# Attention, MLP and routed experts on one core: the routing tables behind the MLP in another order

## The reference

```python
attn = attention(q, k, v)          # B=2, H=8, S=768, D=64; 8 global keys and a local window of 96, ALiBi bias
x = attn.transpose(0, 2, 1, 3).reshape(1536, 512)
h = x @ w_in                       # 512 -> 2048
x = (np.maximum(h, 0) + alpha * np.minimum(h, 0)) @ w_out

logits = x @ w_gate + modality_bias[modality_id]      # 8 experts
e_idx = np.argmax(logits, axis=1)
probs = softmax(logits); gate_w = probs[np.arange(N), e_idx]
for e in range(8):
    mask = e_idx == e
    h = np.maximum(x[mask] @ w1[e], 0.0)              # 512 -> 1024
    out[mask] = gate_w[mask, None] * (h @ w2[e])
```

## Time and profile before

| | us |
|---|---|
| median of 3 runs | 602.53 (600.36 to 602.57) |
| the profiled execution | 599.84 |
| its span | 598.0 |
| mean granted TensorE clock in it | 0.994 of full speed |
| TensorE busy in the span | 582.7 (97%) |
| VectorE, ScalarE, GpSimd busy | 331.0, 187.6, 119.7 |

### The profile page before, as it was taken

The page is one execution under the profiler, slowest core; times in us unless marked ns, Lnnn a source line. Parts: engine busy times, 40 slices in busy tenths (PEclk is TensorE's granted clock), DMA queues, the critical chain, the costliest instruction groups (busy, mean ns, idle before and its releaser), DMA issues.

```text
span 598.0 us, 10696 instructions
## 1 busy us (share of the span) xinstructions
PE 582.7 (97%) x3319; PEld 488.5 (82%) x3320; DVE 331.0 (55%) x846; ACT 187.6 (31%) x435; POOL 119.7 (20%) x187
## 2 busy tenths in 40 slices
PE   8999999999999999999999999999999999999995
PEld 4777777889889989899988999888877887778784
DVE  5877788787644465444554467684221288722211
ACT  4888887342010000100001004131221387521121
POOL 4444443998000000000000000001211112121120
PEclk9999999999999999999999999998999999999998
DMA  7966542463010000100001008015411179211010
GB/s 151 209 135 100 131 124 71 127 193 106 0 54 0 1 1 1 53 0 0 0 0 54 1 2 280 18 54 189 181 53 35 35 238 315 83 52 36 35 52 17
DMA packets 74544, 47.63 MB, mean 80 GB/s; under 512 B 52751, under 2 KB 60943, under 8 KB 74512
## 3 DMA queue, kind: packets, MB, share of 16 engines
q1 hardware_dynamic: 70288, 39.50, 23.8%
q0 software_dynamic: 2480, 7.34, 3.7%
q10 hardware_dynamic: 1744, 0.39, 0.3%
HBM read 40.93 MB, written 7.08 MB: 80 GB/s over the span
## 4 chain that ended last, share of the span: by engine, by line
PE 88%; DVE 5%; issue 3%; ACT 3%; DVEq 1%; ACTq 0%
PE wide L1240 12%; PE wide L1242 11%; PE wide L1241 11%; PE bank L1240 11%; PE bank L1242 11%; PE bank L1241 11%; PE wide L1228 9%; PE bank L1485 4%; PE wide L1465 3%; PE wide L1338 2%; ACT p_sc L515 1%; PE wide L1235 1%; DVE h_act L863 1%; PE bank L1477 1%; DVE h_l L866 1%
## 5 line engine op out<-in xcount | busy, mean ns | idle before, releaser
L863 DVE TENSOR_SCALAR h_act<-bank,alpha_sb 128x384 f32<-128x384 f32 x62 | 38.3, 617 | 108.5 <-PE bank L1242 108.5
L1240 PE MATMUL bank<-x_hl,wts 128*128 (+1 forms) x248 | 85.3, 344 | 0.0
L1242 PE MATMUL bank<-x_hl,wts 128*128 (+1 forms) x248 | 83.6, 337 | 0.0
L1241 PE MATMUL bank<-x_hl,wts 128*128 (+1 forms) x248 | 83.3, 336 | 0.0
L1240 PE MATMUL wide<-wts,h_h 128*128 128x512 f32 x192 | 75.6, 394 | 2.3 <-DVE h_l L866 2.3
L1242 PE MATMUL wide<-wts,h_l 128*128 128x512 f32 x192 | 75.9, 395 | 0.0
L1241 PE MATMUL wide<-wts,h_h 128*128 128x512 f32 x192 | 75.7, 394 | 0.0
L1122 DVE TENSOR_TENSOR hg_l<-wide,hg_h 128x256 fp32r<-128x256 f32 (+1 forms) x45 | 21.7, 510 | 62.3 <-ACT hg_h L603 62.3
L1240 PE MATMUL wide<-wts,hg_h 128*128 (+1 forms) x120 | 51.9, 432 | 1.8 <-DVE hg_l L1122 1.7
L1240 PE MATMUL bank<-wts,xg_h 128*128 (+1 forms) x120 | 49.6, 413 | 0.3 <-DVE xg_l L1115 0.3
L1240 PEld LDWEIGHTS bank<-x_hl,wts 128*128 128x128 f32 x248 | 46.6, 188 | 1.7
(11 more groups left out here) (211 smaller groups left out, 1027.0 us busy)
## 6 DMA issues: line engine op xcount, KB each, us to landing
stage<-in_moe_w SPq DMA_DIRECT2D x32, 512.0 KB, 6.5
ring<-in_moe_w_in SPq DMA_DIRECT2D x16, 256.0 KB, 2.9
ring<-in_moe_w_out SPq DMA_DIRECT2D x16, 256.0 KB, 2.8
v_raw<-in_v SPq DMA_DIRECT2D x16, 192.0 KB, 2.8
x_scratch<-x2row SPq DMA_DIRECT2D x4, 768.0 KB, 4.2
k_raw<-in_k SPq DMA_DIRECT2D x14, 192.0 KB, 3.3
q_raw<-in_q SPq DMA_DIRECT2D x14, 192.0 KB, 3.9
v_win<-in_v SPq DMA_DIRECT2D x16, 96.0 KB, 2.6
```

The source lines that it names most:

```text
L863: link(ts(h, acc, 0.0, alpha_sb[:, j:j + 1], ALU.min, ALU.mult))
L1240: pe.matmul(acc, lhs[0], rhs[0], start=start, stop=False)
L1241: pe.matmul(acc, lhs[0], rhs[1], start=False, stop=False)
L1242: return pe.matmul(acc, lhs[1], rhs[0], start=False, stop=stop)
```

## The change

- DVE's counts and firsts are computed for base alone first; order, and the flags of used experts, come later.
- hi_hot goes away; hi_val is written directly, in two halves of six token groups, each with its own signal; TensorE waits for the second one after six matmuls. hi_val's TensorE product is followed by more of tile 0's filling.
- The first expert's low parts are split from MLP step 11 on (kc 0 to 3, then 4), so three remain for after the group, not five.
- DVE does hidden_low(0, 1) and the table te_f ahead of src_i; tiles_known comes ahead of experts_known.
- The gates' table becomes two fp32r columns per tile (gate_hl: high and low part of the gate), multiplied in one fp32r pass of 40 columns behind everything else, with DVE adding the halves. keep_warm is gone, and turn_x(1) stands ahead of the gates' product.
- TensorE: the three turn_row together (the third into another PSUM tile), the logits of the third row behind one more piece of tile 0. In each tile of the loop `up_first` issues the eight products of xg_h, then the four of xg_l, with the wait for xg_l between them.

```diff
             link(dve.tensor_reduce(counts[:, 0], tmp_s[:], AX_X, ALU.add))
-            link(ts(counts[:, 1], counts[:, 0], 0.0, None, ALU.is_gt))
-            for m in range(2):
-                last_ = tt(tmp_c[:, m], counts[:, m:m + 1].broadcast_to([P, E + 1, E]), ahead[:], ALU.mult)
-            link(last_)
-            link(dve.tensor_reduce(firsts[:], tmp_c[:], AX_X, ALU.add))
+            link(tt(tmp_c[:, 0], counts[:, 0:1].broadcast_to([P, E + 1, E]), ahead[:], ALU.mult))
+            link(dve.tensor_reduce(firsts[:, 0], tmp_c[:, 0], AX_X, ALU.add))
...
+            HT = NT // 2
+            for i0 in (0, HT):
+                h = slice(i0, i0 + HT)
+                spread = lambda x: x.unsqueeze(2).broadcast_to([P, HT, NW])
+                link(tt(hi_val[:, h, 0], iota_s[:].unsqueeze(1).broadcast_to([P, HT, NW]), spread(tpos[:, h]), ALU.is_equal))
+                tt(hi_val[:, h, 1], hi_val[:, h, 0].bitcast(F32), spread(tok_id[:, h]), ALU.mult).then_inc(hi_ready, 1)
+            hidden_low(0, 1)
+            link(ts(counts[:, 1], counts[:, 0], 0.0, None, ALU.is_gt))
+            link(tt(tmp_w[:], iota_s[:].unsqueeze(2).broadcast_to([P, NW, E]),
+                    base[:, 0:E].unsqueeze(1).broadcast_to([P, NW, E]), ALU.is_ge))
+            link(tt(tmp_w[:], tmp_w[:], used.unsqueeze(1).broadcast_to([P, NW, E]), ALU.mult))
+            link(dve.tensor_reduce(te_f[:], tmp_w[:], AX_X, ALU.add))
 
             dve.wait_ge(slots_ready, 1)
...
+            for m in range(2):
+                tt(hi_gate[:, :, m], hi_val[:, :, 0].bitcast(F32),
+                   gate_hl[:, m].bitcast(F32).unsqueeze(2).broadcast_to([P, NT, NW]), ALU.mult).then_inc(hi_ready, 1)
+
+            gathered_low(1)
             dve.wait_ge(slots_ready, 2)
-            dve.tensor_copy(slot_gate[:], banks[0][:, 0:NW]).then_inc(tables_ready, 1)
+            link(dve.tensor_copy(slot_gate[:], wide[1][:, 512 + 2 * NW:512 + 3 * NW]))
+            tt(slot_gate[:], slot_gate[:], wide[1][:, 512 + 3 * NW:512 + 4 * NW], ALU.add).then_inc(tables_ready, 1)
...
+                def up_first(t, o):
+
+                    pe.wait_ge(xg_high, t + 1)
+                    for c in range(DC):
+                        if c % 2 == 0:
+                            pe.wait_ge(e_low, o * KC + c // 2 + 1)
+                        for m in range(2):
+                            pe.matmul(banks[0][:], xg_h[:, c], exp_w(o - 1, c // 2, m)[:, c % 2], start=c == 0 and m == 0, stop=False)
+                    pe.wait_ge(xg_low, t + 1)
+                    for c in range(DC):
+                        last = pe.matmul(banks[0][:], xg_l[:, c], exp_w(o - 1, c // 2, 0)[:, c % 2], start=False, stop=c == DC - 1)
+                    last.then_inc(hA_ready, 1)
...
-                down_part(0, 1, range(4))
+                down_part(0, 1, range(2))
                 turn_h(0, 1)
...
+                down_part(0, 1, range(2, 4))
+                pe.wait_ge(hg_low, 2)
+                down_part(0, 1, range(4, 6))
+                pe.wait_ge(hg_low, 3)
+                down_part(0, 1, range(6, 8))
+                turn_x(1)
+                pe.wait_ge(hi_ready, 4)
                 for i in range(NT):
-                    last = pe.matmul(banks[0][:, 0:NW], lo_hot[:, i].bitcast(F32), hi_gate[:, i],
+                    last = pe.matmul(wide[1][:, 512 + 2 * NW:512 + 4 * NW], lo_hot[:, i], hi_gate[:, i].rearrange("p m s -> p (m s)"),
                                      start=i == 0, stop=i == NT - 1)
                 last.then_inc(slots_ready, 1)
-                pe.wait_ge(hg_low, 2)
-                down_part(0, 1, range(4, 6))
-                keep_warm(2)
-                turn_x(1)
-                pe.wait_ge(hg_low, 3)
-                down_part(0, 1, range(6, 8))
```

More of the change, by code:

```diff
@@ L209, in bass_attention_moe_kernel @@
         yrow = sb("yrow", [P, D])
-        hi_hot = sb("hi_hot", [P, NT, NW])
         hi_val = sb("hi_val", [P, NT, 2, NW], F32R)
-        hi_gate = sb("hi_gate", [P, NT, NW])
+        hi_gate = sb("hi_gate", [P, NT, 2, NW], F32R)
+        gate_hl = sb("gate_hl", [P, 2, NT], F32R)
         tmp_e = sb("tmp_e", [P, NT, E])
@@ L623, in _ @@
                 act.wait_ge(x2_turned, (NG - 1) * GT + a + 1)
-                act.copy(x2T_last[:, a], wide[2][:, a % 2 * 512:a % 2 * 512 + D]).then_inc(x2T_ready, 1)
+                act.copy(x2T_last[:, a], (wide[0] if a == 2 else wide[2])[:, a % 2 * 512:a % 2 * 512 + D]).then_inc(x2T_ready, 1)
             hidden_row(0, 0)
@@ L1019, in group @@
                             dve.tensor_copy(source0[:], wide[1][:, 592:593]).then_inc(source0_ready, 1)
-                        if j in (13, 14):
-                            split_low(0, j - 13)
+                        if 11 <= j <= 14:
+                            split_low(0, j - 11)
                         if j == 15:
                             gathered_low(0)
-                            split_low(0, 2)
+                            split_low(0, 4)
                     elif not first:
@@ L1137, in _ @@
             dve.tensor_copy(x2row[:, 1], wide[0][:, 512:512 + D]).then_inc(x2_middle, 1)
-            for kc in range(3, 7):
+            for kc in range(5, KC):
                 split_low(0, kc)
@@ L1172, in _ @@
             tt(dst_i[:], dst_f[:], slot(1), ALU.add).then_inc(tables_ready, 1)
-            hidden_low(0, 1)
-            split_low(0, 7)
+            tt(new_i[:, 0:NS], te_f[:, 1:NW], te_f[:, 0:NS], ALU.subtract)
+            dve.tensor_copy(te_i[:], te_f[:])
+            link(tt(tmp_c[:, 1], counts[:, 1:2].broadcast_to([P, E + 1, E]), ahead[:], ALU.mult))
+            link(dve.tensor_reduce(firsts[:, 1], tmp_c[:, 1], AX_X, ALU.add))
+            dve.tensor_copy(totals_i[:], firsts[:, :, E]).then_inc(tiles_known, 1)
             link(tt(used_id[:], used, iota_e[:], ALU.mult))
@@ L1331, in turn_row @@
                         pe.wait_ge(x2_copied, 2 * g + (3 if a < 2 else 4))
-                    turn(wide[2][:, a % 2 * 512:a % 2 * 512 + 512], [x2row[:, a, c * P:(c + 1) * P] for c in range(DC)],
+                    dst = wide[0] if isinstance(g, int) and g == NG - 1 and a == 2 else wide[2]
+                    turn(dst[:, a % 2 * 512:a % 2 * 512 + 512], [x2row[:, a, c * P:(c + 1) * P] for c in range(DC)],
                          x2_turned)
@@ L1362, in after_attention @@
                 group(NG - 1, last=True)
-                def keep_warm(n):
-                    for _ in range(n):
-                        pe.matmul(wide[2][:, 512:1024], mlp_w(FC - 1, 0)[:, 0:P], mlp_w(FC - 1, 1), start=True, stop=True)
                 def turn_x(t):
@@ L1394, in down_part @@
                         last.then_inc(y_ready, 1)
+                def up_first(t, o):
[9 more added lines that the diff above has]
+                    last.then_inc(hA_ready, 1)
                 def tile(t, o):
-                    pe.wait_ge(xg_low, t + 1)
-                    up_part(t, o, 0, range(4))
+                    up_first(t, o)
                     up_part(t, o, 1, range(2))
@@ L1416, in after_attention @@
                 up_part(0, 1, 0, [0], x0)
-                turn_row(NG - 1, 0)
-                turn_row(NG - 1, 1)
+                for a in range(GT):
+                    turn_row(NG - 1, a)
                 up_part(0, 1, 0, [1], x0)
                 logits(NG - 1, 0, last_group=True)
-                turn_row(NG - 1, 2)
                 logits(NG - 1, 1, last_group=True)
+                up_part(0, 1, 0, [2], x0)
                 logits(NG - 1, 2, last_group=True)
-                up_part(0, 1, 0, [2, 3], x0)
+                up_part(0, 1, 0, [3], x0)
                 count_experts(NG - 1)
```

16 lines of the change are left out of this document (6 added, 10 removed).

## The result

| | kernel before | changed kernel |
|---|---|---|
| median, us | 601.75 (599.89 to 602.57, 16 runs) | 603.28 (601.92 to 606.67, 16 runs) |
| the profiled execution | 599.84 | 602.81 |
| its span | 598.0 | 601.0 |

The ratio after to before is 1.0034, interval 1.0023 to 1.0045: some 2 us slower, clear of noise but within the half per cent. The forecast was 603.1, out of a sum of +0.6.

A forecast was written before the change was run, and what follows sets the result against it. Two limits were taken: TensorE's own work and gather(2)'s arrival. The loop starts 1.7 us earlier, but gather(2) resumes TensorE 0.6 later: 599.84 + 0.6 = 600.4, plus 2.7 to the median gives 603.1, range 600.3 to 605.0.

The forecast's parts named there:

- a sum of +0.6: Whole execution: TensorE goes on after gather(2) at 419.2 against 418.56, 0.6 us later, and only its own work follows.
- its own sign: Profile behind gather(2)'s wait: the forecast is wrong if the idle is missing or matmuls of 0.43 us spacing follow it.
- rival B: TensorE's wait for gather(2): the clock falls there, costing 1.6 us more, 604.7 as a median; chance 0.15.
- the arrival of gather(2): Second gathered tile's transposes: only about 0.2 us to spare before; now landing at 419.1, TensorE idling over 2 us.
- The gates' product and the low clock at 406 to 410: Ahead of the tile loop: product 1.34 us instead of 2.84, no granted clock below 1.00 in 404 to 410.
- TensorE idles before the counting: Behind the logits: one filling piece instead of two covers choose, so TensorE idles 0.7 us.
- Before the slots' product: Slot values in halves: TensorE idles 0.6 us for the first half, and the product ends 0.2 us earlier.
- idle before turn_x(1): Behind the filling: TensorE idles from 408.1 to 409.0 for gather(1), 0.9 us.
- The tile loop begins: Start of the tile loop: at 410.7 to 411.0 against 412.52, 1.7 us earlier, including 0.3 from xg_l's wait.
- gather(2)'s issue: GpSimd behind slot_gate: issue at 412.0, 0.9 us later than before, with 0.4 taken for loading the number of tiles.
- The flight: gather(2) beside the experts' loads: 7.1 us from issue to landing, against 3.5 alone.
- src_i behind the tiles' table: DVE chain: src_i comes at 404.9 instead of 404.27; the table's instructions would be free behind it.

The follow-up runs named there:

- run 1: Changed kernel with gather(2) issued right behind gather(1), no longer waiting for slot_gate and the load of the number of tiles: 600.2 us, ratio 0.9974.
- run 2: Changed kernel with SP's loads of the next expert begun only when gather(2) has landed: 600.49 us, ratio 0.9981.
- run 3: Kernel before with gather(2) made to wait for tile 0's scaled rows: 604.31 us, ratio 1.0046.
- run 4: Kernel before with the gates' product in one fp32r pass of 20 columns, the gates' low part left out: 600.42 us, ratio 0.9974.
- run 12: Changed kernel with third logits put back, gather(2) right behind gather(1), and up_first replaced by the old product order: 599.48 us, ratio 0.9971.
- run 11: Changed kernel with gather(2) issued ahead of the load of the number of tiles, still behind slot_gate: 602.97 us, ratio 1.0041.
- run 6: Changed kernel with the copy of src_i ahead of the tiles' table: 604.2 us, ratio 1.004.
- run 9: Changed kernel with third logits put back ahead of two filling pieces and gather(2) right behind gather(1): 598.76 us, ratio 0.9961.
- run 5: Changed kernel with the third logits put back ahead of the two filling pieces: 602.53 us, ratio 1.0017.
- run 10: Changed kernel with third logits put back, gather(2) right behind gather(1), and SP's loads behind gather(2)'s landing: 600.19 us, ratio 0.9979.

## Where the prediction was right, and where only its number was

- By its own sign the forecast did not come true: matmuls of 0.43 us spacing stand behind the idle (421.16 and on), and that was the sign for rival B. The time came out at the forecast's number and not at B's 604.7 because two errors cancelled, as worked out below.
- What bounds the kernel: TensorE as the bottleneck, and the arrival of gather(2) as a limit that lay just behind it with 0.2 us to spare, was right. Runs 1 to 3 show it from three sides.
- The gates' product and the low clock at 406 to 410: as forecast, 12 matmuls in one pass, clock 1.00 throughout; run 4 shows the gain by itself (of one fp32r pass, with the gates' low part left out).
- TensorE idles before the counting: 0.54 (forecast 0.7), choose at 395.14 (395.0; the last MLP group itself ended 0.1 later in this profile). Before the slots' product 0.40 (0.6). src_i at 404.97 (404.9). gather(1) lands at 408.7 (408.85), idle before turn_x(1) 0.36 (0.9; part of the forecast's idle went into the later filling). hi_gate ready at 409.05 (408.9).
- The tile loop begins at 411.35, not 410.7 to 411.0. I had let the end of xg_l's wait shorten this; the profile shows 0.65 of "issue" there, time in which TensorE waits for nothing that it shows. In the program two numbers are loaded and a branch is taken there; that these fill the 0.65 is likely, and no run takes them away. With the old product order (run 12) the profile puts 0.57 down to xg_l, but that was ready at 410.84, 0.47 before the loop began at 411.31, so either way 0.5 to 0.65 stand there.
- gather(2)'s issue at 412.44, not 412.0: the load of the number of tiles costs 1.05, and I took 0.4 out of 0 to 1.7. Run 11 measures 1.0. The flight was 7.3 (7.1). TensorE resumed 1.25 late, not 0.6: 0.4 from the issue and 0.2 from the flight. This is the mis-sized term.
- That src_i behind the tiles' table was a loss was wrong: putting it ahead gained nothing (run 6).
- Rival B happened, and I had given it 0.15: the clock fell in the wait for gather(2), 2.0 us after TensorE's last matmul had ended; behind the last matmul of the kernel before it had been 2.5. It costs 1.49 in the profiled execution (B had 1.6), and all 16 executions have one low stretch at least; where it lies is seen in one of them. Forecast and B together make +2.2 for the profiled run; measured is +3.0, by the 0.65 of the later issue and flight and 0.26 further on, less 0.1 for the cheaper stretch.
- That the median still came out at 603.28, 0.2 from the forecast, is luck. I added 2.7, by which the profiled execution lay below the median of three, as if the changed kernel kept that distance. It did not: its profiled execution lies 0.5 below its median. So +0.6 and +2.7 make 3.3 where +3.0 and +0.5 were measured. The 602.53 was high too: 16 runs give 601.75, and by its place in the table it holds two low stretches, where the changed kernel mostly has one. The wait for gather(2) was right as a mechanism and the clock was not; the size was 0.6 instead of 1.5 by the medians (603.28 - 601.75) or 2.0 by the ratio.
- The rules of the Trainium skill that the prediction names ("DMA: Bandwidth & Descriptors", "Anatomy of one DMA" and "Queues, rings and completion order") would have let gather(2) land in time, by the estimate of 3.2 us that it works out from them. The traces disagree with that time: 3.3 to 3.5 us alone, 6.1 to 8.9 beside the loads. Whether the turns between the queues are otherwise than the page says, no view here shows.

## What to carry to other kernels

Before a step is moved that makes a value which a DMA-issuing engine waits for, look at the landing of the next transfers against the moment they are needed, not at the step's own cost: here a gather had 0.2 us of slack, and the 3.1 us between the medians of the changed kernel and of run 1 hang on where it is issued. A transfer that depends only on an index table should not stand behind a wait for anything else, though an earlier issue beside other loads need not land earlier (run 11). Where the clock comes and goes between executions of one kernel, compare executions with as many low stretches, and not one profile with one median. And an instruction that fills a wait is not made free by moving it behind the wait (run 6).

## What the runs showed of the hardware that I had not expected

- An indirect gather of 256 KB flies 3.3 to 3.5 us alone, and 6.1 (runs 1 and 12), 6.8 (run 3), 7.2 (before), 7.3 (changed, run 9), 7.4 (run 4), 7.5 and 7.8 (runs 5 and 6) and 8.9 (run 11) beside eight loads of 512 KB that SyncE began 0.7 to 5.6 us earlier. The spread does not follow the distance to the loads' start (0.66 us: 6.1; 0.81: 7.3; 2.3: 8.9; 3.4: 7.3; 5.6: 6.8), and what sets it stays open.
- Executions of one and the same program differ in the number of low stretches of the granted clock, by 1.2 to 1.7 us each. Thin matmuls or idleness stood before each one seen: the transposes and logits (runs 3, 4 and 10, at 394 to 395), the gates' product and the idle places around it (runs 1 and 11, at 411 to 412), the wait for gather(2) (changed, run 6). In run 5 TensorE waited longer for it, 2.56 us, and the clock fell only 1.0 us behind the wait, at about 420.7. The same instructions at the same places have a fall in some executions and none in others.
- Reading a number from SBUF into a register of GpSimd stood for 1.0 us between a signal and a DMA's issue (run 11 against the changed kernel).
